# Issuing the first logits from two engines, and normalising the first chunk's softmax weights in two halves

## The chip, the cores and the metric

The kernel runs on one core of a Trainium2 chip. The metric is the device time of one execution in microseconds (us): 718.46 us is the median of three runs of the kernel before (718.26 to 718.46). Engines are named as in the profile: PE (TensorE; PEld is its weight load), DVE (VectorE), ACT (ScalarE), POOL (GpSimd) and SP (SyncE, which here only issues DMAs).

## The reference

Two stages. A local attention with seven taps and eight heads makes the input of a gated feed-forward block with a three-tap convolution.

```python
w = exp(weight_gen - max(weight_gen, axis=-1))       # B=4, S=4160, H=8, K=7
w = w / (sum(w, axis=-1) + 1e-9)
x_pad = 6 zero rows ahead of each batch of x         # D=192, group = D // H = 24
x = einsum('bshk,bskhg->bshg', w, x_pad[:, s + k])   # the attention output
h = maximum(x @ w_in, 0)                             # d_ff = 1024
conv_out = sum_k conv_w[k] * h[s + k - 1]            # three taps, along the sequence
out = (h * sigmoid(conv_out)) @ w_out
```

## The kernel before

The four batches form one stream of tokens, cut into 17 chunks of up to 1022 tokens. Partition p of a chunk holds eight consecutive tokens (i = 0 to 7) and their six predecessors, so that the taps are shifts inside a partition. For each chunk: the logits are loaded, their maximum is taken and subtracted (DVE, `maxima` and `subtract_top`), ACT takes the exponential (`exponent`), DVE sums and inverts (`sums`), and `normalise` (L467) writes the weights into `soft`. Then token place by token place the weights are multiplied with the rows of x (`multiply`, L486), the seven taps are summed, the sum is turned onto the channels by PE, and PE multiplies with w_in in a hi and lo split (`product_in`, L930). Relu, convolution, sigmoid and gate follow, and PE multiplies with w_out (`product_out`, L952). The work of all engines is laid out by hand in steps; every engine runs its own queue in program order, and semaphores tie them.

The first chunk (FIRST) has a start of its own, which is where the change lies:

- SP issues, in this order: the logits of FIRST in three pieces (L535; `logit_pieces` gives row 0 with seven tokens, 1.5 KB; rows 1 to 112, 196 KB; rows 113 to 127, 26.2 KB), the x of FIRST in six pieces (L517; three with the first eight rows of each window, "early", on `s_x_early[0]`, and three with the rest, on `s_x[0]`), the logits of chunks 1 and 2, w_in, conv_w, the x of chunk 1 and w_out. The first piece of logits waits on `s_cleared` for DVE's memset of logits (L761), the piece of x that holds row 0 for the memset of x_win (L762).
- ACT loads its function table ahead of its first activation (L740), then does `exponent` of FIRST, `copy_soft` (L658), `exponent` of chunk 1, and the split of w_in.
- DVE does maximum, subtraction, sums and `normalise` of FIRST, then `own_product` of places 1 and 3 (each 1344 elements a partition; they read the copy `soft_own`, which lies in a bank of PSUM), the maximum and subtraction of chunk 1, `own_product` of 5 and 7, the sums of chunk 1, and four sums of taps (L799). POOL does places 0, 2, 4 and 6 from `soft`.
- PE runs 26 warming matmuls (L914, `WARM`, 52 entries in the trace, since each fp32 matmul shows as two), then `sum_and_turn` of places 1, 3, 5 and 7 (L991; it adds the taps in PSUM), the turn of the convolution weights between 3 and 5, the turns of the other places, the low part of w_in, and then the first `product_in`.

Of the kernel before, what the change touches and what calls it, by code (L numbers as in the profile page):

```python
# [7 lines left out]
ALU = mybir.AluOpType  # L8
# [9 lines left out]
SLOTS = 8  # L18
# [8 lines left out]
BY_TENSOR = (1, 3, 5, 7)  # L27
SUMS_FIRST = (0, 2, 4, 6)
FIRST_ROWS = 8
GROUPS = [(0,), (1,), (2,), (3, 4), (5, 6, 7, 8, 9), (10, 11, 12, 13, 14), (15, 16)]  # L30
GROUP_SLOTS = 5
EXPONENT = 6
# [60 lines left out]
def local_attention_gated_expert(nc, x, weight_gen, w_in, conv_w, w_out, masks, out):  # L93
# [208 lines left out]
    with ExitStack() as ctx:  # L302
# [58 lines left out]
        s_inverse = sem("s_inverse")  # L361
        s_norm = sem("s_norm")
        s_soft = sem("s_soft")
        s_soft_own = sem("s_soft_own")
        s_weighted = sem("s_weighted")
        s_weighted_dve = sem("s_weighted_dve")
# [24 lines left out]
        attn_first = gated[0:FIRST.parts, len(BY_VECTOR), 0:TOKENS * D].rearrange("p (i d) -> p i d", d=D)  # L391
        soft_bank = z[2][:, 1, :]
        soft_own = soft_bank[0:FIRST.parts, 0:FIRST.tokens * HK]

        def places(c, i, count):

# [103 lines left out]
        def logits_landed(c):  # L500

            return 16 * sum(len(logit_pieces(d)) for d in CHUNKS if d.number <= c.number and slot_of(d) == slot_of(c))

        block = ctx.enter_context(nc.Block())

        @block.sync
        def _(sp):
            def load_x(c):
                if c.number >= 2:
                    before = CHUNKS[c.number - 2]  # L510
                    sp.wait_ge(s_weighted, products_before(before, before.tokens))
                    if before is FIRST:
                        sp.wait_ge(s_weighted_dve, len(BY_VECTOR))
                for a, b, offset, n, row in x_pieces(c):
                    if a == 0 and c is FIRST:
                        sp.wait_ge(s_cleared, 2)
                    sp.dma_start(x_win[a:b, c.ring, offset * D:(offset + n) * D],  # L517
                                 bass.AP(x_flat.tensor, row * D, [[c.tokens * D, b - a], [1, n * D]])) \
                        .then_inc(s_x_early[c.number] if c in CHUNKS[:2] and offset < FIRST_ROWS else s_x[c.ring], 16)

            def load_mask(c):
                place = MASKED.index(c)
                if place >= 2:
                    sp.wait_ge(s_soft, MASKED[place - 2].number + 1)
                sp.dma_start(mask[:, place % 2, :],
                             bass.AP(masks.tensor, c.number * (P * TOKENS * K), [[TOKENS * K, P], [1, TOKENS * K]])) \
                    .then_inc(s_mask[place % 2], 16)

            def load_logits(c):
                if c.number >= GROUP_SLOTS:  # L530
                    sp.wait_ge(s_exp, GROUPS.index(group_of(CHUNKS[c.number - GROUP_SLOTS])) + 1)
                for a, b, offset, n, row in logit_pieces(c):
                    if offset and a == 0 and c is FIRST:
                        sp.wait_ge(s_cleared, 1)
                    sp.dma_start(logits[a:b, slot_of(c), offset * HK:(offset + n) * HK],  # L535
                                 bass.AP(w_flat.tensor, row * HK, [[c.tokens * HK, b - a], [1, n * HK]])) \
                        .then_inc(s_logits[slot_of(c)], 16)

            def store(t):
                c, v = TILES[t]  # L540
                sp.wait_ge(s_out_sb, t + 2)
                for a, b, row in store_pieces(t):
                    sp.dma_start(bass.AP(out_flat.tensor, row * D, [[D, b - a], [1, D]]), out_sb[a:b, t % OUTS, :]) \
                        .then_inc(s_store[t % OUTS], 16)

            def load_weights():
                sp.dma_start(stage_a, w_in[0:P, :]).then_inc(s_weights, 16)
                sp.dma_start(stage_b[0:D2, :], w_in[P:D, :]).then_inc(s_weights, 16)
                sp.dma_start(conv_rows, conv_w.rearrange("t (j p) -> (t j) p", p=P)).then_inc(s_conv_rows, 16)

            load_logits(FIRST)
            load_x(FIRST)
            for c in CHUNKS[1:3]:
                load_logits(c)
            load_weights()
            for c in CHUNKS[1:2]:
                if c in MASKED:
                    load_mask(c)
            load_x(CHUNKS[1])
            sp.dma_start(wo[:, :, :], w_out.rearrange("(j p) d -> p j d", p=P)).then_inc(s_weights_out, 16)  # L560
            for k in range(FIRST_STEP, LAST_STEP + 1):
                for c in CHUNKS[2:]:
                    if group_of(c) in GROUPS[3:] and k == top_at(c) - 6:
                        load_logits(c)
                    if k == start_of(c) - 10:
                        if c in MASKED:
                            load_mask(c)
                        load_x(c)
                if k - 1 in TILE_STEP:
                    store(TILE_STEP[k - 1])  # L570
            for t in range(FIRST_LAST_TILE, len(TILES)):
                store(t)
            for r in range(OUTS):

                sp.wait_ge(s_store[r], 16 * (1 + sum(len(store_pieces(t)) for t in range(r, len(TILES), OUTS))))

        @block.gpsimd
        def _(pool):
            nc.gpsimd.memset(ident[:, :], 0.0).then_inc(s_ident, 1)
            pool.wait_ge(s_ident, 1)  # L580
            nc.gpsimd.affine_select(out=ident[:, :], in_=ident[:, :], compare_op=ALU.not_equal, fill=1.0,
                                    base=0, pattern=[[-1, P]], channel_multiplier=1).then_inc(s_ident, 1)

            def product(c, i):
                if i == 0:
                    pool.wait_ge(s_soft, c.number + 1)
                if i == 0 or c in CHUNKS[:2]:
                    wait_x(pool, c, i)
                if c is not FIRST and i % 2 == 0 and place_of(c, i) >= RING - 1:
                    pool.wait_ge(s_attn, summed_before(place_of(c, i) + 2 - RING))  # L590
                multiply(nc.gpsimd, c, i, soft).then_inc(s_weighted, 1)

            def normalise_next(c):

                pool.wait_ge(s_weighted, products_before(c, c.tokens))
                if c is FIRST:
                    pool.wait_ge(s_soft_own, 1)
                normalise(pool, nc.gpsimd, CHUNKS[c.number + 1])

            def apply_gate(n):  # L600
                c = chunk_of(n)
                pool.wait_ge(s_gate, n + 1)
                nc.gpsimd.tensor_tensor(gated_flat(c, n), gated_flat(c, n), hidden[:, n % 3, 1:1 + c.size], ALU.mult) \  # L603
                    .then_inc(s_gated_pool, 1)

            def step(k):
                for c, i in SUM_AT.get(k + AHEAD, []):
                    product(c, i)
                    if i == TOKENS - 1 and c is not LAST:
                        normalise_next(c)  # L610
                for c in CHUNKS[2:]:
                    if group_of(c) in GROUPS[3:] and k == top_at(c) + 1:
                        pool.wait_ge(s_top, c.number + 1)
                        subtract_top(nc.gpsimd, c)
                n = STEP_OF.get(k - 1)
                if n is not None and on_pool(n):
                    apply_gate(n)

            for i in range(FIRST.tokens):
                if i not in BY_VECTOR:  # L620
                    product(FIRST, i)
            normalise_next(FIRST)
            for k in range(FIRST_STEP, LAST_STEP + 1):
                step(k)

        @block.scalar
        def _(act):
# [26 lines left out]

            def copy_soft():

                act.wait_ge(s_soft, 1)
                nc.scalar.copy(soft_own, soft[0:FIRST.parts, 0:FIRST.tokens * HK]).then_inc(s_soft_own, 1)  # L658

            def exponent(g):  # L660
                f, l = CHUNKS[g[0]], CHUNKS[g[-1]]
# [55 lines left out]
            def step(k):  # L717
# [18 lines left out]
                if k in EXPONENT_AT:  # L736
                    exponent(EXPONENT_AT[k])

            act.wait_ge(s_ident, 2)
            nc.scalar.activation(minus, ident[:, :], ACT.Copy, scale=-1.0).then_inc(s_minus, 1)  # L740
            exponent(GROUPS[0])
# [18 lines left out]
        def _(dve):  # L760
# [21 lines left out]
            def apply_gate(n):  # L782
                c = chunk_of(n)
                dve.wait_ge(s_gate, n + 1)
                nc.vector.tensor_tensor(gated_banks(c, n), shifted(c, n, 1), conv(c, n), ALU.mult).then_inc(s_gated, 1)

            def own_product(c, i):
                dve.wait_ge(s_soft_own, 1)
                wait_x(dve, c, i)
                multiply(nc.vector, c, i, soft_own).then_inc(s_weighted_dve, 1)  # L790

            def sum_taps(c, i):
                first = i - i % 2
# [77 lines left out]
            def attention_first():  # L871
                c = FIRST
                shift(c)
                sums(c)
                normalise(dve, nc.vector, c)
                for i in BY_VECTOR[:2]:
                    own_product(c, i)
                shift(CHUNKS[1])
# [207 lines left out]
```

## Time and profile before

| | us |
|---|---|
| median of three runs | 718.46 |
| the profiled execution, device time | 718.5 |
| its span, first to last instruction | 716.7 |
| PE busy | 706.4 (99%) |
| DVE busy | 614.3 (86%) |
| POOL busy | 614.2 (86%) |
| ACT busy | 497.3 (69%) |
| granted TensorE clock, mean | 1.00 |

1.8 us of the profiled execution lie outside its span. Times in the rows are us from the start of the span. A row of a timeline gives the start, the busy time, the engine, the line, the operation, what it writes and reads, its shape and how many were merged into the row; in brackets stands how long the engine was idle ahead of it and what ended that. The chain of waits is followed back from the last instruction. "SPq" is SP's queue of DMA issues: its durations are those of the issue, not of the transfer.

### The profile page before, as it was taken

How to read it: one execution, taken by the hardware profiler on the slowest of the kernel's cores; microseconds unless marked ns; L12 is line 12 of the kernel's file. 1: busy time of each engine (PE TensorE's matmuls, PEld its weight loads, DVE VectorE, ACT ScalarE, POOL GpSimd, SP SyncE). 2: the span in 40 equal slices, each digit the busy share in tenths (PEclk: the TensorE clock that was granted, in tenths of full speed). 3: DMA queues.
4: the chain of work that ended last, by engine and by line, in shares of the span. 5: the costliest groups of instructions: out<-in, count | busy, mean ns of one | idle time of the engine just before them, and what ended most of it. 6: DMA issues, size and time to landing. Idle time of an engine off the chain costs nothing.

```text
span 716.7 us, 9863 instructions
## 1 busy us (share of the span) xinstructions
PE 706.4 (99%) x3839; PEld 634.6 (89%) x3839; DVE 614.3 (86%) x549; ACT 497.3 (69%) x636; POOL 614.2 (86%) x285
## 2 busy tenths in 40 slices
PE   8997999999999999999999999999999999999998
PEld 8756889899999999999989898989899999999997
DVE  7998999999988989898898989898999989885630
ACT  3658867696767676776977676677777867676641
POOL 5999999999997999999899999989898899925310
PEclk9999999999999999999999999999999999999999
DMA  8420312103031222212030210203020200000001
GB/s 239 145 104 1 91 51 77 44 22 100 18 100 30 72 60 55 86 36 95 23 101 16 69 50 23 93 23 108 27 93 23 50 21 20 23 18 23 23 29 34
DMA packets 26297, 41.44 MB, mean 58 GB/s; under 512 B 3864, under 2 KB 23678, under 8 KB 24461
## 3 DMA queue, kind: packets, MB, share of 16 engines
q1 hardware_dynamic: 26250, 40.81, 18.7%
q8 instruction: 30, 0.49, 0.3%
q14 instruction: 17, 0.14, 0.1%
HBM read 28.02 MB, written 12.78 MB: 57 GB/s over the span
## 4 chain that ended last, share of the span: by engine, by line
PE 95%; ACT 2%; DVE 2%; issue 0%; DMA 0%; SPq 0%; ACTq 0%
PE out_ps L952 45%; PE z L930 41%; PE turn_ps L974 3%; PE turn_ps L952 2%; PE z L942 1%; PE z L991 1%; PE turn_ps L991 0%; PE out_ps L991 0%; ACT hidden L634 0%; PE z L952 0%; DVE z L773 0%; DVE z L779 0%; ACT gated L653 0%; DMA logits<-in_weight_gen 0%; DVE xb L824 0%
## 5 line engine op out<-in xcount | busy, mean ns | idle before, releaser
L486 POOL TENSOR_TENSOR weighted<-x_win,soft 128x1344 f32<-128x1344 f32 (+1 forms) x128 | 351.1, 2764 | 7.4 <-DMA x_win<-in_x 7.3
L952 PE MATMUL out_ps<-wo,gated 128*128 128x192 f32 x2000 | 346.0, 326 | 0.2
L952 PEld LDWEIGHTS out_ps<-wo,gated 128*128 128x128 f32 x2000 | 326.9, 190 | 8.4 <-ACT out_sb L689 0.8
L603 POOL TENSOR_TENSOR gated<-gated,hidden 128x1022 f32<-128x1022 f32 (+1 forms) x117 | 248.4, 2123 | 73.9 <-ACT gated L653 73.7
L773 DVE SCALAR_TENSOR_TENSOR z<-hidden,cw,z 128x1022 f32<-128x1022 f32 (+1 forms) x134 | 164.6, 1229 | 59.8 <-ACT z L640 59.0
L634 ACT ACTIVATE hidden<-z 128x1024 f32<-128x1024 f32 (+1 forms) x136 | 134.5, 989 | 106.5 <-PE z L930 99.0
L779 DVE SCALAR_TENSOR_TENSOR z<-hidden,cw,z 128x1022 f32<-128x1022 f32 (+1 forms) x134 | 166.2, 1240 | 4.2
L640 ACT ACTIVATE z<-hidden,cw 128x1022 f32<-128x1022 f32 (+1 forms) x134 | 144.9, 1081 | 4.2
L814 DVE TENSOR_REDUCE attn_a<-weighted 128x256 f32<-128x1792 f32 (+1 forms) x62 | 124.8, 2012 | 0.0
L653 ACT ACTIVATE gated<-z 128x1022 f32<-128x1022 f32 (+1 forms) x117 | 115.1, 984 | 12.0 <-PE out_ps L952 7.1
L930 PE MATMUL z<-xa_hi,wa_hi 128*128 128x512 f32 (+1 forms) x264 | 100.1, 458 | 5.4 <-ACT gated L653 5.2
L930 PE MATMUL z<-xa_hi,wa_lo 128*128 128x512 f32 (+1 forms) x264 | 83.2, 394 | 0.0
L930 PE MATMUL z<-xb,wb_hi 128*128 128x512 f32 (+1 forms) x264 | 82.7, 392 | 0.0
L930 PE MATMUL z<-xb,wb_lo 128*128 128x512 f32 (+1 forms) x264 | 82.6, 391 | 0.0
L930 PE MATMUL z<-xa_lo,wa_hi 128*128 128x512 f32 (+1 forms) x264 | 82.4, 390 | 0.0
L814 DVE TENSOR_REDUCE attn_b<-weighted 128x128 f32<-128x896 f32 (+1 forms) x62 | 67.0, 1080 | 0.7
L930 PEld LDWEIGHTS z<-xb,wb_hi 128*128 128x128 f32 x264 | 49.9, 189 | 11.6
L930 PEld LDWEIGHTS z<-xb,wb_lo 128*128 128x128 f32 x264 | 49.6, 188 | 11.5 <-ACT wb_lo L702 0.2
L930 PEld LDWEIGHTS z<-xa_hi,wa_lo 128*128 128x128 f32 x264 | 49.6, 188 | 11.1
L930 PEld LDWEIGHTS z<-xa_lo,wa_hi 128*128 128x128 f32 x264 | 49.6, 188 | 11.0
L930 PEld LDWEIGHTS z<-xa_hi,wa_hi 128*128 128x128 f32 x264 | 46.4, 190 | 8.3 <-ACT gated L653 4.4
L689 ACT COPY out_sb<-out_ps 128x192 f32<-128x192 f32 x125 | 38.9, 311 | 14.5 <-PE out_ps L952 14.5
(83 smaller groups left out, 394.6 us busy)
## 6 DMA issues: line engine op xcount, KB each, us to landing
x_win<-in_x SPq DMA_DIRECT2D x11, 1344.0 KB, 6.4
out<-out_sb SPq DMA_DIRECT2D x111, 96.0 KB
logits<-in_weight_gen SPq DMA_DIRECT2D x12, 224.0 KB
x_win<-in_x SPq DMA_DIRECT2D x2, 1008.0 KB
out<-out_sb SPq DMA_DIRECT2D x16, 84.0 KB
x_win<-in_x SPq DMA_DIRECT2D x1, 1176.0 KB
x_win<-in_x SPq DMA_DIRECT2D x1, 768.0 KB, 10.1
wo<-in_moe_w_out SPq DMA_DIRECT2D x1, 768.0 KB, 13.9
```

The source lines that it names most:

```text
L486: return engine.tensor_tensor(to, rows, s, ALU.mult)
L603: nc.gpsimd.tensor_tensor(gated_flat(c, n), gated_flat(c, n), hidden[:, n % 3, 1:1 + c.size], ALU.mult) \
L634: nc.scalar.activation(hidden[:, n % 3, 0:c.cols].rearrange("p (a b) -> p a b", a=c.banks), z[n % 3][:, 0:c.banks, 0:c.cols // c.banks], A ...
L640: nc.scalar.activation(conv(c, n), shifted(c, n, 1), ACT.Copy, scale=cw[:, 1, n % J:n % J + 1]) \
L653: nc.scalar.activation(to, conv(c, n), ACT.Sigmoid).then_inc(s_gate, 1)
L689: nc.scalar.copy(out_sb[0:rows, t % OUTS, :], bank[0:rows, 0:D]).then_inc(s_out_sb, 1)
L773: nc.vector.scalar_tensor_tensor(out=conv(c, n), in0=shifted(c, n, 0), scalar=cw[:, 0, n % J:n % J + 1], in1=conv(c, n), op0=ALU.mult, op1 ...
L779: nc.vector.scalar_tensor_tensor(out=conv(c, n), in0=shifted(c, n, 2), scalar=cw[:, 2, n % J:n % J + 1], in1=conv(c, n), op0=ALU.mult, op1 ...
L814: nc.vector.tensor_reduce(to, products, AX.X, ALU.add).then_inc(s_attn, 1)
L930: last = nc.tensor.matmul(z[n % 3][:, bank, 0:width], weights, moving[:, bank * width:(bank + 1) * width], start=(m == 0), stop=(m == len( ...
L952: last = nc.tensor.matmul(bank[0:end - begin, 0:D], gated[:, j, begin:end], wo[:, j, :], start=(j == 0), stop=(j == J - 1))
L974: last = nc.tensor.transpose(bank_of(c, r)[:, at * c.parts:(at + 1) * c.parts], src, ident[0:c.parts, 0:c.parts])
```

## The change

It has two parts. First, SP issues only the large piece of FIRST's logits and goes on to x; the pieces with row 0 and with rows 113 to 127 are issued by ACT at the head of its queue, ahead of the activation of L740, and the wait on `s_cleared` goes to ACT with them. Second, DVE normalises FIRST's weights in two instructions, tokens 0 to 3 and tokens 4 to 7 (`normalise_first`), with a semaphore for the first (`s_soft_half`); ACT copies each half when it is there, the second half into another bank (`soft_own_late`, in `z[0]`). DVE's products of 1 and 3 wait for the first copy, those of 5 and 7 for the second; POOL's products of 0 and 2 wait for the first half, those of 4 and 6 for both. The other chunks are untouched.

```diff
+FIRST_LOGITS = 1
+        soft_own_late = z[0][0:FIRST.parts, 1, 0:FIRST.tokens * HK]
+        def load_first_logits(eng, engine, pieces):
+            for a, b, offset, n, row in pieces:
+                if offset and a == 0:
+                    eng.wait_ge(s_cleared, 1)
+                engine.dma_start(logits[a:b, 0, offset * HK:(offset + n) * HK],
+                                 bass.AP(w_flat.tensor, row * HK, [[FIRST.tokens * HK, b - a], [1, n * HK]])) \
+                    .then_inc(s_logits[0], 16)
 # SP
-                    if offset and a == 0 and c is FIRST:
-                        sp.wait_ge(s_cleared, 1)
-            load_logits(FIRST)
+            load_first_logits(sp, nc.sync, logit_pieces(FIRST)[FIRST_LOGITS:FIRST_LOGITS + 1])
             load_x(FIRST)
 # POOL
             def product(c, i):
-                if i == 0:
+                if c is FIRST and i < c.half:
+                    pool.wait_ge(s_soft_half, 1)
+                elif c is FIRST or i == 0:
                     pool.wait_ge(s_soft, c.number + 1)
 ...
-                    pool.wait_ge(s_soft_own, 1)
+                    pool.wait_ge(s_soft_own, 2)
 # ACT
             def copy_soft():
+                half = FIRST.half * HK
+                act.wait_ge(s_soft_half, 1)
+                nc.scalar.copy(soft_own[:, 0:half], soft[0:FIRST.parts, 0:half]).then_inc(s_soft_own, 1)
                 act.wait_ge(s_soft, 1)
-                nc.scalar.copy(soft_own, soft[0:FIRST.parts, 0:FIRST.tokens * HK]).then_inc(s_soft_own, 1)
+                nc.scalar.copy(soft_own_late[:, half:2 * half], soft[0:FIRST.parts, half:2 * half]).then_inc(s_soft_own, 1)
 ...
+            load_first_logits(act, nc.scalar, logit_pieces(FIRST)[:FIRST_LOGITS] + logit_pieces(FIRST)[FIRST_LOGITS + 1:])
             act.wait_ge(s_ident, 2)
             nc.scalar.activation(minus, ident[:, :], ACT.Copy, scale=-1.0).then_inc(s_minus, 1)
 # DVE
+            def normalise_first(part):
+                c = FIRST
+                tokens = slice(part * c.half, (part + 1) * c.half)
+                if part == 0:
+                    dve.wait_ge(s_inverse, 1)
 ...
+                nc.vector.tensor_tensor(to, e, r, ALU.mult).then_inc(s_soft_half if part == 0 else s_soft, 1)
             def own_product(c, i):
-                dve.wait_ge(s_soft_own, 1)
+                dve.wait_ge(s_soft_own, 1 if i < c.half else 2)
                 wait_x(dve, c, i)
-                multiply(nc.vector, c, i, soft_own).then_inc(s_weighted_dve, 1)
+                multiply(nc.vector, c, i, soft_own if i < c.half else soft_own_late).then_inc(s_weighted_dve, 1)
 ...
-                normalise(dve, nc.vector, c)
+                normalise_first(0)
+                normalise_first(1)
```

## Rows read from the trace of the kernel before

**Rows 1.** Chain of waits, 0 to 60 us: start, us, what.
```profile
0.94 0.34 SPq L535
1.71 2.38 DMA logits<-in_weight_gen
10.53 1.83 PE turn_ps L991 x14
54.98 0.59 ACT xa_hi L680
```

**Rows 2.** The page's part 4: the chain by engine, shares of the span.
```profile
PE 95%; ACT 2%; DVE 2%; issue 0%; DMA 0%; SPq 0%; ACTq 0%
```

**Rows 3.** Timeline of PE, 5 to 17 us.
```profile
4.88 4.97 PE L914 MATMUL z<-ident 128*128 128x128 f32 x37
10.53 1.83 PE L991 MATMUL turn_ps<-ident,gated 128*128 128x128 f32 x14 [0.68 <-DVE gated L486]
13.76 1.73 PE L991 MATMUL turn_ps<-ident,gated 128*128 128x128 f32 x14
```

**Rows 4.** Timeline of DVE, 1 to 17 us.
```profile
1.14 1.18 DVE L762 MEMSET x_win<- 1x1344 f32 x1 [0.23 <-issue]
...
4.12 0.62 DVE L829 TENSOR_REDUCE top<-logits 128x64 f32<-128x448 f32 x1 [1.18 <-DMA logits<-in_weight_gen]
...
7.35 0.97 DVE L467 TENSOR_TENSOR soft<-expo,inverse 128x448 f32<-128x448 f32 x1
8.92 1.55 DVE L486 TENSOR_TENSOR gated<-x_win,z 128x1344 f32<-128x1344 f32 x1 [0.60 <-ACT z L658]
11.16 1.55 DVE L486 TENSOR_TENSOR gated<-x_win,z 128x1344 f32<-128x1344 f32 x1 [0.69 <-DMA x_win<-in_x]
...
13.29 0.62 DVE L458 TENSOR_TENSOR logits<-logits,z 128x448 f32<-128x448 f32 x1
13.83 3.01 DVE L486 TENSOR_TENSOR gated<-x_win,z 128x1344 f32<-128x1344 f32 x2
```

**Rows 5.** Timeline of SP's DMA issues, 1.7 to 3.3 us.
```profile
1.71 0.42 SPq L535 DMA_DIRECT2D logits<-in_weight_gen  x1
...
2.18 0.39 SPq L517 DMA_DIRECT2D x_win<-in_x  x1
...
3.08 0.25 SPq L517 DMA_DIRECT2D x_win<-in_x  x1
```

**Rows 6.** Waits of SP's queue, 0 to 32 us: total, times, longest.
```profile
SPq L1077 <- PEq L1077: 0.7, 1, 0.7
SPq L535 <- DVE logits L761: 0.2, 1, 0.2
```

**Rows 7.** Busy time by stretch: PE, PEld, DVE, ACT, POOL; PEclk, DMA share, GB/s.
```profile
2.30:3.20 0.90, 0.90 (x7) 0.90 (x6) 0.35 (x7) 0.03 (x1) 0.00 (x0) 1.00 0.72 227
3.20:3.90 0.70, 0.70 (x5) 0.70 (x5) 0.00 (x0) 0.00 (x0) 0.00 (x0) 1.00 0.66 102
...
5.50:8.60 3.10, 3.10 (x27) 3.10 (x26) 2.21 (x3) 0.76 (x2) 0.00 (x0) 1.00 1.00 243
```

**Rows 8.** Timeline of ACT, 0 to 40 us.
```profile
0.73 1.28 ACT L740 ACT_TABLE_LOAD   x1 [0.73 <-PEq L1077]
...
5.43 0.58 ACT L674 ACTIVATE expo<-logits 128x448 f32<-128x448 f32 x1 [3.09 <-DVE logits L458]
8.35 0.54 ACT L658 COPY z<-soft 128x448 f32<-128x448 f32 x1 [2.34 <-DVE soft L467]
...
23.91 0.58 ACT L680 CAST xa_hi<-turn_ps 128x512 fp32r<-128x512 f32 x1 [3.13 <-PE turn_ps L974]
...
26.32 1.01 ACT L702 CAST wa_lo<-z 128x1024 fp32r<-128x1024 f32 x1 [1.21 <-PE z L1016]
...
35.37 1.28 ACT L653 ACT_TABLE_LOAD   x1
```

**Rows 9.** Timeline of POOL, 8 to 19 us.
```profile
8.74 10.29 POOL L486 TENSOR_TENSOR weighted<-x_win,soft 128x1344 f32<-128x1344 f32 x4 [7.28 <-DMA x_win<-in_x]
```

More of the change, by code:

```diff
@@ L363, in local_attention_gated_expert @@
         s_soft = sem("s_soft")
+        s_soft_half = sem("s_soft_half")
         s_soft_own = sem("s_soft_own")
@@ L785, in apply_gate @@
                 nc.vector.tensor_tensor(gated_banks(c, n), shifted(c, n, 1), conv(c, n), ALU.mult).then_inc(s_gated, 1)
+            def normalise_first(part):
[3 more added lines that the diff above has]
+                    dve.wait_ge(s_inverse, 1)
+                e = expo[0:c.parts, 0, 0:c.tokens * H * SLOTS].rearrange("p (i h s) -> p i h s", i=c.tokens, s=SLOTS)[:, tokens, :, 0:K]
+                r = inverse[0:c.parts, 0, 0:c.tokens * H].rearrange("p (i h) -> p i h", i=c.tokens)[:, tokens, :].unsqueeze(3) \
+                    .to_broadcast([c.parts, c.half, H, K])
+                to = soft[0:c.parts, 0:c.tokens * HK].rearrange("p (i k h) -> p i h k", i=c.tokens, k=K)[:, tokens]
+                nc.vector.tensor_tensor(to, e, r, ALU.mult).then_inc(s_soft_half if part == 0 else s_soft, 1)
             def own_product(c, i):
-                dve.wait_ge(s_soft_own, 1)
+                dve.wait_ge(s_soft_own, 1 if i < c.half else 2)
                 wait_x(dve, c, i)
-                multiply(nc.vector, c, i, soft_own).then_inc(s_weighted_dve, 1)
+                multiply(nc.vector, c, i, soft_own if i < c.half else soft_own_late).then_inc(s_weighted_dve, 1)
             def sum_taps(c, i):
```

## The prediction

> **What bounds the kernel now.** I read the chain of waits first. By engine it is PE for 95% of the span [rows 2]: after the start PE is the engine that has no time to spare, and whatever shortens the kernel must let PE's string of matmuls begin earlier, or run shorter. The change touches only the first 17 us or so. So the next view is the chain from 0 to 60 us. It goes from SP's first issue at 0.94 to the third one, whose transfer lands at 1.71 + 2.38 = 4.09 [rows 1], through DVE's maximum, which stood idle for 1.18 us until then [rows 4], down to DVE's normalisation at 7.35, ACT's copy at 8.35 and DVE's product of place 1 from 8.92 to 10.47 [rows 4, 8]; at 10.53 PE begins `sum_and_turn` [rows 1, 3]. From there the chain stays on PE, but for short steps, until it hands over to ACT at 54.98 [rows 1].
>
> The third view is PE's own timeline. The warming matmuls end at 4.88 + 4.97 = 9.85, and PE then stands idle for 0.68 us until the product of place 1 is there [rows 3]. This is the number that matters most: the change leaves the warming matmuls as they are, so PE cannot start `sum_and_turn` before about 9.85, whatever is gained ahead of it. **The cap is 10.53 - 9.85 = 0.68 us.**
>
> **The change, part by part.** I write L for the landing of the last piece of FIRST's logits (before: 4.09) and follow it to PE.
>
> *The issue on SP.* SP was free at 0.7 and stood for 0.2 us for the memset of logits [rows 6]; its issues of logits began at 0.94, and the x issues at 2.18 [rows 1, 5]. Now its one piece of logits waits for nothing: it goes out at about 0.75, and with about 0.35 us an issue, x follows at about 1.1, that is 1.1 us earlier. The large piece alone was the second issue (about 1.3); it gains about 0.55 us. The x piece with row 0, the third of x, was issued at 3.08 [rows 5]; it waits for the memset of x_win, over at 1.14 + 1.18 = 2.32 [rows 4], so it and all behind it on SP gain 3.08 - 2.35 = 0.7 us. Everything behind (logits of chunks 1 and 2, w_in, conv_w, x of chunk 1, w_out) moves up by that and arrives no later.
>
> *The issue on ACT.* Two issues, at 0.94 (the memset is waited for as before) and about 1.33, by SP's durations of 0.34 to 0.42 [rows 1, 5]. Behind them on ACT are the table load of 1.28 us, the small activation, and the exponential, before which ACT was idle for 3.09 us [rows 8]. The 0.8 us of issues is hidden in that idle time; without that cover it would cost its 0.8 us.
>
> *The landing.* The last piece, rows 113 to 127, is issued at 1.33 instead of 1.71. With the same 2.38 us to landing [rows 1], L = 3.71. But x now follows the large piece directly, while before the first x came 0.5 us after the last logits [rows 5] and the DMA engines had room: they were busy for 0.72 and 0.66 of the time from 2.30 to 3.90 [rows 7]. The 26 KB piece now lies in the midst of x traffic. No row shows an issue on ACT, nor two queues at once. Bounds: 3.4 (the piece no longer has 196 KB ahead of it in its own queue; 196 KB at the 227 GB/s of [rows 7] are 0.9 us, and I allow a third of that), and 3.71 + 0.9 = 4.6 (as much x traffic comes between as the large piece took). I take 3.9, nearer to the unchanged 2.38 us, since that is the only duration that a row has.
>
> *From L to the normalisation.* Untouched: 7.35 - 4.09 = 3.26 us [rows 1, 4].
>
> *Two halves.* The normalisation took 0.97 us for 448 elements, where an ordinary one of 448 took 0.62 and one of 1344 took 1.55 [rows 4]. The last two give (1.55 - 0.62) / 896 = 1.04 ns an element and 0.155 us fixed, so the normalisation costs (0.97 - 0.155) / 448 = 1.82 ns an element, and a half of 224 costs 0.155 + 0.41 = 0.56 us. Two instructions that don't wait for each other overlap by 3.10 - 3.01 = 0.09 us [rows 4], so the pair takes 1.03 to 1.15 us; I take 1.05, which is 0.08 us more of DVE. ACT's copy: 0.54 us for 448 and 1.01 for 1024 [rows 8], so 0.82 ns an element, 0.17 fixed, and 0.36 for a half. The first copy is done 0.56 + 0.02 + 0.36 + 0.02 = 0.96 us after the normalisation began, under the second half. So the copy is off the path: the product of place 1 begins 1.05 us after the normalisation does (at most 1.18), instead of 8.92 - 7.35 = 1.57. That is 0.5 us gained (0.4 to 0.55). The second copy runs on ACT beside DVE's product; ACT has nothing else there.
>
> *The product of place 1* therefore begins at L + 3.26 + 1.05 = L + 4.31, ends 1.55 later, and PE could begin 0.06 after that: L + 5.92. With L = 3.9 that is 9.82, just before the warming matmuls end. PE begins at 9.85. **Gain 0.68 us.** With L unchanged (4.09) it would be 10.01, 0.52 gained; with 4.6 it is 10.52, nothing gained.
>
> *Is x there?* POOL's first product began at 8.74, and it waited for x, not for the weights [rows 9]; so the early x landed shortly before. The stream now begins 0.55 us earlier and without the gap of 3.2 to 3.9 [rows 7]: I take 8.0 (7.5 to 8.7). DVE wants it at 8.2. If x doesn't move at all, the product ends at 10.25 and 0.2 us is gained. The rest of x bound DVE's product of place 3, at 11.16 [rows 4]. Is that what is late next? PE needs this product when it is through place 1: 9.85 + (13.76 - 10.53) = 13.1 [rows 3]. Unmoved it ends at 12.71: not late, even then. Places 5 and 7 were there at 13.83 + 3.01 = 16.84 [rows 4]. PE takes 3.23 / 2 = 1.6 us for half a place, and wants the last product after five of those, at about 17.9. POOL starts 0.6 to 0.7 earlier, with x.
>
> *Behind it.* ACT, before its first take of turned data, was idle for 3.13 us until PE was there [rows 8], so the weights' splitting isn't in the way and all follow PE. POOL, with 10.29 us of products [rows 9], follows x. I expect 0.68 us to arrive at the end undiminished: the profiled execution would be 718.5 - 0.7 = 717.8, and the median, which it equals within 0.04, 718.46 - 0.68 = 717.8 us.
>
> **Rule and row.** On the arbitration of the queues, the Trainium skill (DMA: Bandwidth & Descriptors, Queues, rings and completion order) says that SP and ACT each own a ring on the same DMA engines, that an engine takes packets from its rings in turn, and that a completion increment lands only after every earlier write of that engine across its queues. The trace of before has one queue only and can't show it. It speaks against this change: the completion of ACT's small pieces would wait for x packets that before stood behind it. The same page (Issuing engines are not separate DMA queues) says that issuing from several engines saves only the sequencer's time; that is how the sum above treats it.
>
> **Rivals.**
>
> *Small pieces held back by x.* The small piece is taken in turn with x and completes behind it. For: x follows within 0.4 us and keeps the DMA engines busy throughout, as at 5.50 to 8.60 [rows 7]. Against: only 15 rows and one are concerned. L between 4.1 and 4.6: PE at 10.0 to 10.5, a gain of 0 to 0.5, say 718.2 us. This is the page's rule, taken as a mechanism of this kernel. Chance 0.2.
>
> *Slower.* The same contention, carried further: from L = 4.6 on the path is longer than before. If the piece lands at 5.3, PE begins at 11.2 and the kernel takes 719.1 us; if it came only with the whole early x, at 8.0, PE would begin at 13.9 and the time would be 721.8. L must be 6.05 for 0.2%. Chance 0.08, of it 0.03 beyond 0.2%.
>
> *ACT issues late.* If the table load stood ahead of the issues, they would go out at 2.0 and 2.4 [rows 8], L = 4.8, PE at 10.7: 718.65 us. Both table loads of the trace stand right ahead of the activation that needs them, though, the second at 35.37 [rows 8]. Chance 0.06.
>
> *Gain lost on the way.* The chain leaves PE at 54.98 for ACT [rows 1]; if POOL or DVE had moved up less than PE, part of it would be kept there: 718.1 us. Chance 0.1.
>
> **How the numbers follow.** The forecast has 0.53, and about 0.03 is left for a gain above the cap, through a happier order later. It is 717.8 us. The range takes in the gain of the cap and 0.35 for such shifts below, and above it the held back piece and the late issue: 717.4 to 718.7. 0.2% of 718.46 is 1.44 us, about what can be told from no change for this kernel; it needs twice the cap to be faster by that, and L past 6 to be slower. Faster 0.04, same 0.92, slower 0.04.
>
> **What the profile will show.** Right if: SP's first x issue is near 1.1; ACT's issues come ahead of its table load; DVE's maximum starts at about 3.9; the normalisation shows as two of 0.56; the product of place 1 starts at about 8.2 with no wait for ACT; and PE goes from the warming matmuls to `sum_and_turn` without idle time. Wrong if the maximum starts after 4.3, if PE still stands idle ahead of L991, or if the first `product_in` has moved but the end has not.

## The result, and the profile after

The changed kernel takes 723.49 us (median of four runs, 722.47 to 723.61) against 718.46: a ratio of 1.0067 with a 95% interval of 1.0055 to 1.0080. It is 5.0 us slower, where 717.8 was forecast with a range of 717.4 to 718.7. The profiled execution took 723.46 us with a span of 721.7, so 1.8 us lie outside the span as before, and the whole loss is inside it.

The chain of waits of the changed kernel, 0 to 80 us (start, us, what), to be read beside [rows 1]:

```profile
0.94 0.51 ACTq L512
...
1.48 5.55 DMA logits<-in_weight_gen
...
12.87 3.35 PE turn_ps L1020 x14
16.22 2.76 PE out_ps L1020 x14
18.98 1.56 PE turn_ps L1020 x14
...
34.38 7.31 PE z L959 x30
```

Two things stand in it. ACT's second issue, at 1.48, landed 5.55 us later, at 7.03, where the last piece had landed at 4.09 [rows 1]. And the first 28 entries of `sum_and_turn` took 3.35 + 2.76 = 6.1 us, where the next 28 went at 1.56 us for 14, which is 3.1. The timelines of the same kernel (SP's queue, ACT, DVE, PE), beside [rows 3 to 5, 8]:

```profile
1.18 0.41 SPq L529 DMA_DIRECT2D x_win<-in_x  x1
...
2.34 0.23 SPq L529 DMA_DIRECT2D x_win<-in_x  x1
...
1.85 1.28 ACT L756 ACT_TABLE_LOAD   x1 [1.85 <-DVE logits L777]
...
7.06 0.62 DVE L857 TENSOR_REDUCE top<-logits 128x64 f32<-128x448 f32 x1 [4.13 <-DMA logits<-in_weight_gen]
...
10.29 0.96 DVE L813 TENSOR_TENSOR soft<-expo,inverse 128x224 f32<-128x224 f32 x2
...
11.26 3.02 DVE L489 TENSOR_TENSOR gated<-x_win,z 128x1344 f32<-128x1344 f32 x2
...
1.52 7.70 PE L943 MATMUL z<-ident 128*128 128x128 f32 x52 [1.52 <-POOL ident L591]
...
12.87 3.35 PE L1020 MATMUL turn_ps<-ident,gated 128*128 128x128 f32 x14 [3.65 <-DVE gated L489]
```

The change does what it says: x goes out at 1.18 (2.18 before, [rows 5]), the table load stands behind ACT's issues, the two halves take 0.96 us together, and the product of place 1 follows them at once and waits for nothing. Only the logits are late. PE, done with its warming at 9.22, stands idle for 3.65 us, and in that time its granted clock falls. Busy time by stretch of the same kernel, PE alone (PE, PEclk, DMA share, GB/s):

```profile
9.30:12.80 3.50, 0.00 (x0) 0.85 1.06 300
12.90:19.00 6.10, 6.10 (x30) 0.53 0.89 312
19.00:22.00 3.00, 3.00 (x28) 1.00 0.00 0
```

From 12.9 to 19.0 the granted clock was 0.53, the lower level (1.2 GHz) nearly throughout, and 30 entries fitted in 6.1 us; then 28 went in 3.0 us at the upper one (2.4 GHz). So the 5.06 us by which the first `product_in` came later (34.38 against 29.32 in the chain of before) are 12.87 - 10.53 = 2.34 us of later start and 21.51 - 18.79 = 2.72 us of slower matmuls between the two points.

### The profile page after: what moved, and what is told of

It is laid out like the page before. It is cut to its first block, busy times and chain, and to the rows that moved or that the text cites. A ratio compares the mean times of both kernels' runs of the same rounds, so it can differ in the third digit from the quotient of the medians.

```text
span 721.7 us, 9868 instructions
## 1 busy us (share of the span) xinstructions
PE 708.4 (98%) x3839; PEld 636.7 (88%) x3839; DVE 614.3 (85%) x550; ACT 497.3 (69%) x637; POOL 614.1 (85%) x285
## 4 chain that ended last, share of the span: by engine, by line
PE 94%; DVE 2%; ACT 2%; DMA 1%; issue 1%; ACTq 0%
PE out_ps L981 45%; PE z L959 41%; PE turn_ps L1003 3%; PE turn_ps L981 2%; PE z L971 1%; PE z L1020 1%; DMA logits<-in_weight_gen 1%; PE turn_ps L1020 1%; PE out_ps L1020 1%; ACT hidden L646 0%; PE z L981 0%; DVE z L789 0%; DVE z L795 0%; ACT gated L665 0%; DVE xb L852 0%
```

## The experiments

One table holds the numbers on which the verdicts rest: the first issue of x, the start of DVE's first maximum (just behind the last landing of the logits), PE's idle time ahead of `sum_and_turn` and its start, the start of the first `product_in` in the chain, the span, all of the profiled execution, and the median of the runs with the ratio to the kernel before and its interval.

| kernel | x issued | maximum | PE idle | PE starts | product_in | span | median | ratio (95%) |
|---|---|---|---|---|---|---|---|---|
| before | 2.18 | 4.12 | 0.68 | 10.53 | 29.32 | 716.7 | 718.46 | |
| changed | 1.18 | 7.06 | 3.65 | 12.87 | 34.38 | 721.7 | 723.49 | 1.0067 (1.0055 to 1.0080) |
| e1 halves only | 2.18 | 4.13 | 0.72 | 10.37 | 29.16 | 716.5 | 718.33 | 0.9997 (0.9988 to 1.0006) |
| e2 issue only | 1.19 | 7.16 | 3.71 | 13.55 | 33.74 | 721.0 | 723.89 | 1.0073 (1.0059 to 1.0086) |
| e3 x behind logits | 3.59 | 3.60 | 1.28 | 11.01 | 29.80 | 717.1 | 718.90 | 1.0008 (0.9999 to 1.0017) |
| e4 42 warming | 1.19 | 6.99 | none | 13.02 | 31.70 | 719.1 | 721.31 | 1.0038 (1.0025 to 1.0052) |
| e5 one x piece ahead | 1.18 | 6.18 | 3.06 | 12.00 | 33.64 | 721.0 | 722.22 | 1.0044 (1.0029 to 1.0059) |
| e6 x behind memset | 2.34 | 3.51 | none | 9.93 | 28.62 | 715.9 | 717.69 | 0.9988 (0.9979 to 0.9997) |
| e7 large first, SP | 1.91 | 3.52 | none | 10.29 | 28.98 | 716.3 | 717.48 | 0.9988 (0.9979 to 0.9997) |
| e8 row 0 on ACT | 1.70 | 3.46 | none | 10.12 | 28.81 | 716.2 | 717.80 | 0.9991 (0.9982 to 1.0000) |
| e9 e7, 22 warming | 1.90 | 3.51 | none | 9.62 | 28.41 | 715.7 | 717.53 | 0.9988 (0.9979 to 0.9997) |
| e10 e7, whole | 1.92 | 3.48 | none | 9.95 | 28.75 | 716.2 | 717.98 | 0.9994 (0.9985 to 1.0003) |
| e11 x behind conv_w | 1.66 | 3.72 | none | 9.87 | 28.56 | 716.0 | 717.85 | 0.9994 (0.9985 to 1.0003) |
| e12 e8, 22 warming | 1.69 | 3.46 | 0.31 | 9.79 | 28.58 | 716.0 | 717.52 | 0.9985 (0.9976 to 0.9994) |

A first reading: in all 14 kernels the span less the start of the first `product_in` is 687.3 to 687.5 us. Nothing of the start is given back or added later; what happens up to that point is the whole matter.

**Which half of the change?** e1 keeps the two halves and gives all logits back to SP:

```diff
-            load_first_logits(sp, nc.sync, logit_pieces(FIRST)[FIRST_LOGITS:FIRST_LOGITS + 1])
+            load_first_logits(sp, nc.sync, logit_pieces(FIRST))
-            load_first_logits(act, nc.scalar, logit_pieces(FIRST)[:FIRST_LOGITS] + logit_pieces(FIRST)[FIRST_LOGITS + 1:])
```

> The normalisation in two halves with its two copies, and SP issues all three pieces of the first logits as in the kernel before. If the loss of 5 us comes from the issue on ACT alone, the logits land at 4.09 as before, the product of place 1 starts near 8.4 instead of 8.92, PE starts sum_and_turn near 10.0 instead of 10.53, and the time is 0.5 us below the kernel before, 717.9 us. If the halves are part of the loss (POOL's early start beside DVE's second half, or the second bank), the time is above 718.5.

Measured 718.33 us (11 runs), no difference that can be told from before, so the forecast of 717.9 was not borne out; PE started at 10.37, not 10.0. DVE's row for place 1, and POOL's for place 0:

```profile
8.76 1.55 DVE L489 TENSOR_TENSOR gated<-x_win,z 128x1344 f32<-128x1344 f32 x1 [0.42 <-ACT z L673]
...
8.80 10.33 POOL L489 TENSOR_TENSOR weighted<-x_win,soft 128x1344 f32<-128x1344 f32 x4 [7.33 <-DMA x_win<-in_x]
```

The bracket of DVE's row names ACT's second copy, L673, which this product doesn't wait for; the first had ended at 8.32 (7.97 + 0.35 in ACT's timeline). POOL's row, 0.04 us later, names what both waited for: early x. So the halves had the weights ready 0.6 us earlier (at 8.34, where the product started at 8.92 [rows 4]), and x, which landed shortly before 8.74 [rows 9] and no earlier here, took back 0.4 us of it. The loss isn't theirs.

e2 is the other half: ACT's issues, with the normalisation and its copy whole as in the kernel before.

```diff
-                normalise_first(0)
-                normalise_first(1)
+                normalise(dve, nc.vector, c)
```

> ACT issues the two small pieces and SP goes on to x; the normalisation is in one piece as before. Landing theory: the logits land near 7.0 as in the changed kernel, the product of place 1 starts 1.57 us after the normalisation instead of 1.0, PE starts near 13.4, and the time is 0.5 us above the changed kernel, 724.0 us. If the loss needs both parts, it is near 718.5.

Measured 723.89 us, the maximum at 7.16: the whole loss is in the issue. In the profiled execution PE started 0.7 us later than in the changed kernel, and yet the first `product_in` came 0.6 us earlier (33.74 against 34.38), since only 14 entries ran at the low clock (3.22 us) where the changed kernel had about twice as many (3.35 + 2.76 us). That execution, at 722.87 us with a mean clock of 0.998, was the fastest of four; the others, at 0.995, took 723.69 to 724.38, on average 0.5 above the changed kernel's executions at 0.995 (723.46 to 723.61), as forecast.

**ACT's queue by itself, or x beside it?** e3 lets ACT issue as in the changed kernel but holds x back:

```diff
+            sp.wait_ge(s_logits[0], 16 * len(logit_pieces(FIRST)))
             load_x(FIRST)
```

> The changed kernel, but SP waits for all of the first logits to land before it issues x. Theory A (the small pieces are held up by x traffic that the other queue now has beside them): without x beside them they land near 1.48 + 2.38 = 3.9, and the maximum starts there. Theory B (an issue on ACT's queue takes 5.5 us to land by itself): the maximum starts near 7.0 as in the changed kernel. The time as a whole is no measure here, since x comes later: under A the early x lands near 4.0 + 6.4 = 10.4 and PE starts near 12.

The chain of waits of e3, and PE's timeline:

```profile
0.94 0.52 ACTq L512
...
1.49 2.08 DMA logits<-in_weight_gen
...
11.01 1.83 PE L1021 MATMUL turn_ps<-ident,gated 128*128 128x128 f32 x14 [1.28 <-DVE gated L489]
```

2.08 us from issue to landing on ACT's queue, less than the 2.38 of SP's third issue [rows 1]: theory B falls. An issue on ACT, with nothing beside it, lands as fast as one on SP; x beside it made the 5.55. (x itself came sooner than I expected: DVE's product began at 9.40 and PE at 11.01, not near 12, and the kernel took 718.90 us.) Of x, e5 lets one piece of 672 KB go and holds the others until the logits are there:

```diff
                         .then_inc(s_x_early[c.number] if c in CHUNKS[:2] and offset < FIRST_ROWS else s_x[c.ring], 16)
+                    if c is FIRST and (a, b, offset) == x_pieces(c)[0][:3]:
+                        sp.wait_ge(s_logits[0], 16 * len(logit_pieces(FIRST)))
```

> The changed kernel, but SP issues only the first piece of x (rows 1 to 112, early, 672 KB) and then waits for the logits before it goes on. If any x traffic ahead holds ACT's small pieces back until that traffic is through (672 KB at about 300 GB/s from 2.5 are 2.3 us, and 0.7 us to the increment), the logits land at 5.5 to 6.5; if all of the early and later x is needed to make it 7.0, they land well before, at 4 to 4.5; if each small packet only takes one turn beside x, they land at 4.0.

The maximum started at 6.18, inside what the first reading expects: one piece is enough for most of the delay, and more than one turn beside x. The view of DMA queues shows it packet by packet. Changed kernel, three stretches, 2.0 to 3.3, 3.3 to 4.4 and 4.4 to 6.5 us (q1 is SP's queue, q10 ACT's, 32 packets in all; packets, MB, share of the 16 engines):

```profile
q1 hardware_dynamic: 151, 0.40, 96.2%
q10 hardware_dynamic: 2, 0.00, 0.4%
...
q1 hardware_dynamic: 62, 0.38, 98.8%
q10 hardware_dynamic: 4, 0.00, 0.9%
...
q1 hardware_dynamic: 118, 0.44, 93.4%
q10 hardware_dynamic: 26, 0.02, 5.8%
```

**When does x have to come?** e6 delays x until the memset of x_win, e11 only by one small load:

```diff
 # e6
+            sp.wait_ge(s_cleared, 2)
             load_x(FIRST)
 # e11
+            sp.dma_start(conv_rows, conv_w.rearrange("t (j p) -> (t j) p", p=P)).then_inc(s_conv_rows, 16)
             load_x(FIRST)
...
-                sp.dma_start(conv_rows, conv_w.rearrange("t (j p) -> (t j) p", p=P)).then_inc(s_conv_rows, 16)
```

> The changed kernel, but SP waits for the memset of x_win (over at 2.3) ahead of all of x, so that the first x is issued at 2.34 as in the kernel before (2.18) and ACT's pieces have 0.86 us more of a start on it. Theory: x data flow from about 3.4 on, the small pieces are through by 3.0, and the logits land at 3.6; early x lands near 8.7 as before and is then what the product of place 1 waits for: PE starts near 10.4 and the time is 718.3. Rival (the small pieces are late whatever x does once it is issued before they land): logits at 5 or later, and 720 us or more.

> The changed kernel with SP's load of conv_w (12 KB, 24 rows) moved between the large piece of logits and x. The first x is issued near 1.7 instead of 1.18, that is 0.2 us after ACT's second issue (1.48) instead of 0.3 us before it. If what counts is that x data are in the DMA engines' other queue when the small packets come (2.4 to 2.5), x data now come at about 2.7 and the logits land between 3.5 and 5; if the small pieces need to be through (3.0) before x, they still land past 5.

Timelines of e11 (SP's queue, ACT's queue, DVE), and its packets from 2.0 to 3.3 us:

```profile
1.66 2.28 SPq L529 DMA_DIRECT2D x_win<-in_x  x6
...
0.94 0.88 ACTq L512 DMA_DIRECT2D logits<-in_weight_gen  x2
...
3.72 0.62 DVE L857 TENSOR_REDUCE top<-logits 128x64 f32<-128x448 f32 x1 [0.79 <-DMA logits<-in_weight_gen]
...
q1 hardware_dynamic: 163, 0.27, 86.1%
q10 hardware_dynamic: 32, 0.03, 6.8%
```

All 32 packets were through by 3.3. Between an x issue at 1.18 and one at 1.66, with ACT's second issue near 1.48 in both, lie 3.3 us of landing time (7.03 against 3.70): nearer to a switch than to a slope. What decides, by these two kernels, is whether x data are in the engines when the small packets come; that e11 also has 12 KB of conv_w ahead of x was not tried apart. e6 says the same with a longer lead (3.51), and is, at 717.69 us, 0.7 us faster than the kernel before. There early x held the product of place 1 until 8.08, well before the 8.7 that I had expected; it was issued 0.16 us later than in the kernel before and yet came earlier, so PE started at 9.93, not 10.4, and the forecast of 718.3 was 0.6 too high. DVE's timeline of e6:

```profile
8.08 1.55 DVE L489 TENSOR_TENSOR gated<-x_win,z 128x1344 f32<-128x1344 f32 x1 [0.36 <-DMA x_win<-in_x]
```

**The clock.** e4 keeps PE busy until the product is there:

```diff
-WARM = 26
+WARM = 42
```

> The changed kernel with 42 instead of 26 warming matmuls, so that PE is busy until just before the first product is there. Nothing else moves: the logits land near 7.0 and PE starts sum_and_turn near 12.9. Theory: PE's idle stretch of 3.65 us brought its granted clock down, and the first 28 entries of sum_and_turn then took 6.1 us instead of 3.1; with the warming prolonged they take about 3.2 and the time falls by about 2.7 us to 720.8. Rival: the clock falls for another reason (the lone stretch after it), and the time stays at 723.5.

The stretch of the changed kernel that had 0.53, in e4:

```profile
12.90:19.00 6.10, 6.10 (x57) 1.00 0.89 314
```

57 entries instead of 30, clock 1.00, and `product_in` at 31.70 instead of 34.38: 2.68 us back, though the logits were as late (6.99). The median fell by 2.2 us rather than 2.7; the profiled execution of e4 (720.87) is the fastest of its four (to 721.73). The idle time is the cause of the low clock: with PE kept busy it stayed away. In e3 1.28 us of idle time brought none (53 entries in 6.0 us from 11 to 17 us, the full pace), 3.06 us in e5's profiled execution did. It doesn't come every time, though. Of e5's four executions two had a mean clock of 0.995 (722.76 and 722.96 us), one 0.998 (721.68) and one 1.000 (720.06): the same kernel with and without the price, which is 2.7 to 2.9 us. Nor is a short wait always free of it: single executions of the kernel before (720.45 and 720.50, of 21 and 33) and of e3 (720.65, of 10) had 0.998 and were about 2 us longer than the rest; none of them has a trace.

**What the change wanted, without its price.** e7 has everything on SP, the large piece first, so that nothing waits for the memset ahead of it, and keeps the two halves; e8 leaves ACT row 0 alone.

```diff
 # e7
+            pieces = logit_pieces(FIRST)
+            load_first_logits(sp, nc.sync, pieces[1:2] + pieces[0:1] + pieces[2:3])
 # e8
+            load_first_logits(sp, nc.sync, logit_pieces(FIRST)[1:])
...
+            load_first_logits(act, nc.scalar, logit_pieces(FIRST)[:1])
```

> SP issues all logits again, but the large piece first, which needs no memset, then row 0, then rows 113 to 127, then x; nothing on ACT; two halves as in the changed kernel. One queue, so no piece is overtaken: logits land near 1.5 + 2.1 = 3.6 to 3.8, x is issued at 1.9 instead of 2.18 and early x lands 0.3 us earlier, at 8.3; that is what binds the product of place 1. PE starts at about 10.05, the time is 0.5 us below the kernel before: 717.9.

> The changed kernel, but SP issues rows 113 to 127 too, right behind the large piece, and ACT issues row 0 alone. The 26 KB piece is then in the same queue as x and ahead of it: lands near 3.3. Row 0 is one packet of 1.5 KB that was at the DMA engine at 2.8 in the changed kernel, before x was in full flow. If the loss is x overtaking packets of the other queue, this kernel escapes it: logits at 3.4 to 3.7, x issued at 1.55, early x at about 7.8, PE at 9.6 to 9.9, time 717.7. If anything on ACT's queue is held back, row 0 too comes late, and the time is 720 us or more.

Timelines of e7, PE and DVE:

```profile
1.52 8.94 PE L943 MATMUL z<-ident 128*128 128x128 f32 x52 [1.52 <-POOL ident L592]
10.29 1.73 PE L1020 MATMUL turn_ps<-ident,gated 128*128 128x128 f32 x14
...
7.72 1.55 DVE L489 TENSOR_TENSOR gated<-x_win,z 128x1344 f32<-128x1344 f32 x1
```

e7 takes 717.48 us, 0.9 below the kernel before, of which the ratio leaves 0.2 to 1.5 as its interval. The product of place 1 was there at 9.27, and PE went from the warming to `sum_and_turn` without idle time. e8 escapes too, at 717.80: one packet of row 0 is let through while the large piece is in the other queue. Against e7 ACT's issue earned nothing that can be told.

Next, then, is the warming. e9 and e12 are e7 and e8 with `WARM = 22`; e10 is e7 with the normalisation whole (the diff of e2).

> The kernel with the large piece first on SP, in two halves, with 22 instead of 26 warming matmuls. In it the product of place 1 was there at 9.3, and PE came from the warming only at 10.46 (by the chain), so the warming is what ends last. Four matmuls fewer at 0.22 us are 0.9 us: PE starts at 9.5, the time is 0.8 us lower, 716.7. Place 3 is needed at 9.5 + 3.1 = 12.6 and was there at 11.6. Rival: with less warming the clock comes up no later, but another wait (x for place 3) takes over, and nothing is gained: 717.5.

> The kernel with row 0 alone on ACT, in two halves, with 22 warming matmuls: the product of place 1 was there at 9.3 and the warming ended at 10.29, so PE starts at 9.4 to 9.5 and the time falls from 717.8 by 0.8 to 717.0. It and the one with the large piece first tell whether ACT's issue has a worth of its own once the warming no longer hides it: by their first x (1.70 against 1.91) at most 0.2 us.

> The kernel with the large piece first on SP, 26 warming matmuls, but the normalisation and its copy in one piece as in the kernel before. The product of place 1 then starts near 6.75 + 1.57 = 8.3 instead of 7.7 and ends at 9.9, still before the warming's end at 10.3. So the halves are worth nothing here: the time is that of the same kernel with halves, 717.5. If the halves are worth their 0.5 us, it is 718.0.

Timelines of e9, PE and DVE:

```profile
1.52 8.03 PE L943 MATMUL z<-ident 128*128 128x128 f32 x44 [1.52 <-POOL ident L592]
9.62 1.83 PE L1020 MATMUL turn_ps<-ident,gated 128*128 128x128 f32 x14
...
8.01 1.55 DVE L489 TENSOR_TENSOR gated<-x_win,z 128x1344 f32<-128x1344 f32 x1 [0.30 <-DMA x_win<-in_x]
```

In the profiled executions PE started 0.67 us earlier in e9 than in e7 and 0.33 earlier in e12 than in e8. The medians don't follow: 717.53 against 717.48, and 717.52 against 717.80, with runs that scatter by 0.4 to 0.9 us. The forecasts, 716.7 for e9 and 717.0 for e12, both missed. The profiled execution of e7 is no typical one: at 718.07 us it is 0.6 above that kernel's median and among its slowest (717.22 to 718.09), while e9's is its median. Both profiled executions came up to pace late (at 7.56 and 7.53 us, see the last section). As nothing is lost or gained behind the start, a median execution of e7 will have started PE 0.6 us earlier than 10.29, near 9.7 (an estimate), and had hardly anything to gain from less warming. With the warming shortened, early x is the wait again, for the 0.30 us of the row. e10, with 717.5 forecast if the halves are worth nothing there and 718.0 if they are worth their 0.5 us, came out at 717.98: 0.5 above e7, but the two intervals overlap and its profiled execution started PE at 9.95, ahead of e7's 10.29. What the halves are worth, between nothing and 0.5 us, stays open.

## Why the prediction was wrong

**The landing: this term failed.** I took 3.9 us for L, with 3.4 to 4.6 as bounds. It was 7.03. The upper bound charged the small piece with as much x traffic as its own large neighbour had been; the packets show that some 1.2 MB of SP's queue went by instead (0.40 + 0.38 + 0.44 MB from 2.0 to 6.5 us, part of the large piece of logits among them). The row on which the choice rested, 2.38 us from issue to landing, was of a queue with nothing beside it, and e3 shows that it held under that condition (2.08). My statement that no row showed two queues at once was right, and it should have opened the upper bound to the whole of early x, 8.0, which I had only in a rival.

**The rival was right in its mechanism.** "Slower" named the contention and the point from which it decides, L = 4.6. Its sum gives L + 5.92 = 12.95 for PE's start with L = 7.03; it was 12.87. It had a chance of 0.08, though; the reason given against a held back piece (only 16 rows are concerned) was no reason, since the last packet counts and not their number.
**Right:** 3.26 us from L to the normalisation (10.29 - 7.03 = 3.26); 1.05 from there to the product of place 1 (0.97); the pair of halves itself 0.96 against 1.05; x's first and third issue (1.18 and 2.34 against 1.1 and 2.35); the table load behind ACT's issues; all on ACT hidden; no loss or gain behind the first `product_in`. One reading was off without consequence: PE wants the product of place 7 after six half places, not five, so later than the 17.9 given.

**Partly right: the cap.** PE did become bound by its warming as soon as nothing else was late (e6, e7, e8, e10, e11). But the warming's end is no fixed point. I took 9.85 from one execution, and it was at 8.94 to 10.46 in the others with 26 matmuls.

## What to carry to other kernels

A small transfer that something waits for should not be put on another queue beside a large one that starts earlier: here, in one queue ahead of the large one, it cost its issue of 0.4 us, and beside it 3 us. If it must go there, hold the large one back until the small one is on its way: e6 did so with one wait and was 5.8 us faster than the changed kernel. Before a wait is lengthened by an uncertain amount, look at what PE does meanwhile: a few tenths of idle time mostly cost themselves, three more microseconds here cost up to twice that through the clock. And if an operand that two engines wait for gets faster, read both engines' rows for the other operand first; here x was there only 0.2 us ahead of the weights (8.74 and 8.92) and kept most of what the halves gained.

## What the runs showed of the hardware

The delay between the two queues has a sharp edge: x issued 0.3 us ahead of ACT's second issue gives a landing at 7.0, x issued 0.2 us behind it gives 3.7. Why a 1.8 KB packet lets dozens of larger ones pass was not shown. That each engine first runs through its share of the piece that came first would fit the counts (103 of 112 rows of x ahead of the bulk of ACT's) and e5, where one piece alone makes 4.68 us of the 5.55. But the trace doesn't name the engine of a packet, and whether ACT's packets waited in the engines or had not reached them yet was not tested.

The warming matmuls come up to their pace at a different time in each execution. The view gives both stretches below a granted clock of 1.00; the first is of the kernel before, the second of the changed one (PE, PEclk, DMA share, GB/s):

```profile
5.00:7.00 2.00, 2.00 (x14) 1.00 1.01 265
```

```profile
5.00:7.00 2.00, 2.00 (x20) 1.00 0.99 225
```

Up to 5 us both had done 16 entries; in the next 2 us one did 14 and the other 20. Entry by entry, the starts lie 0.21 us apart up to 6.29 us in the kernel before and 0.11 us from there on; that change comes at 4.37 us in e5, 4.96 in the changed kernel and 7.56 in e7. At just these times the trace's record of the granted clock begins, with the upper level (2.4 GHz). Ahead of it nothing is recorded, and the view puts 1.00 there, so that this 1.00 is no measurement. Since 0.21 us is twice 0.11, and is also the pace that the changed kernel had at the lower level from 12.9 us on, the warming most likely ran at 1.2 GHz until the record begins; that is inferred. The traces of e1 and e3 hold no such record at all, and their clock has to be read from the pace. So the same 52 entries took 7.42 us (e5) to 8.94 us (e7), which alone moves PE's start by up to 1.5 us where the warming is what ends last.
